# Gathered rows of expert tiles turned by VectorE in 32x32 blocks and moved on chip, in place of TensorE's transposes

## The chip, the cores and the metric

The kernel runs on one core of one Trainium2 chip. The metric is the device time of one execution in microseconds; the lower the better. A run of this kernel repeats to about 0.1%.

## The reference

Three layers follow one another, all in fp32: attention with a decay, a feed-forward layer with softplus, and a mixture of experts in which every token goes to two of eight experts. Only the last one is touched by the change.

```python
def _moe2_ref(x, w_gate, w_noise, noise, w1, w2):      # x 2304x512, w1 8x512x1024, w2 8x1024x512
    logits = x @ w_gate
    noise_scale = np.log1p(np.exp(x @ w_noise))
    noisy_logits = logits + noise_scale * noise
    top2 = np.argpartition(-noisy_logits, 2, axis=1)[:, :2]
    top2_l = np.take_along_axis(noisy_logits, top2, axis=1)
    top2_l = top2_l - top2_l.max(-1, keepdims=True)
    top2_w = np.exp(top2_l)
    top2_w /= top2_w.sum(-1, keepdims=True) + 1e-09
    out = np.zeros((N, D), dtype=np.float32)
    for e in range(E):
        for k in range(2):
            mask = top2[:, k] == e
            if not mask.any():
                continue
            h = np.maximum(x[mask] @ w1[e], 0.0)
            out[mask] += top2_w[mask, k, None] * (h @ w2[e])
    return out
```

## The kernel before

The first half of the time goes to attention and the feed-forward layer; the change leaves both alone. The expert layer then works through tiles of 128 tokens of one expert each. There are 41 tiles here, numbered g from 0, in slots s = g mod 2. How many tiles an expert has is known only when the kernel runs, so all engines read small tables (`tab`, `tab2`) with the row numbers, the expert of each tile, and whether a quarter of the next expert's weights is due in this tile.

One step g of the loop, engine by engine, in program order:

- **TensorE** (`step` in the tensor block) turns the hidden values of tile g (`hidden_transpose`, L935, 8 transposes of 128x128), computes the first product of tile g+1 (`expert_in`, 24 matmuls), turns the gathered rows of tile g+2 (`tile_transpose`, L881, 4 transposes), and computes the second product of tile g (`expert_out`, 24 matmuls). Every product is made of three matmuls (L789, L790, L791), because each operand is split into a high part and a remainder.
- **ScalarE** makes the high parts: of the hidden values (`split_hidden`, L1213, 2 instructions), of up to two quarters of weights for product one (`split_weights(g + 1, 0)`, L1226), of the turned rows (`split_tile`, L1195), the relu (L1204, L1205), and up to two quarters of weights for product two (`split_weights(g, 1)`). It also issues the small loads of the row lists (L367).
- **VectorE** makes the remainders in the same order (L1604, L1773, L1594, L1773), then scales and adds the result of tile g to the rows fetched from the output (`add_output`, L1616).
- **GpSimd** gathers the rows of tile g+3 (`gather_x`, L598), fetches the output rows of tile g (`old_rows`, L608), which waits until the rows of tile g-1 have landed, and sends the rows of tile g (`send_rows`, L614).
- **SyncE** loads a quarter of an expert's weights (1 MB, `load_raw`, L480) into `raw` as soon as VectorE has split the quarter that lay there.

Each expert but the first two has four quarters to be split, within the two or three steps around its predecessor's first tile. Experts with few tiles bring these splits close together: from 735 to 777 us of the span, three steps in a row hold eight of them.

Of the kernel before, what the change touches and what calls it, by code (L numbers as in the profile page):

```python
# [19 lines left out]
F32 = mybir.dt.float32  # L20
# [7 lines left out]
P = 128  # L28
# [82 lines left out]
def build(nc, qT, kT, kN, vN, w_ff, w_gn, noise, w_ex, c_q, c_k, c_dec, c_sq, c_small, c_pad, out):  # L111
    with ExitStack() as ctx:
# [65 lines left out]
        hE_hi, a = place("hE_hi", [P, FT2, P], F32R, a)  # L178
        hE_lo0, a = place("hE_lo0", [P, FT2 // 2, P], F32R, a)
        hE_lo1, hE_end = place("hE_lo1", [P, FT2 // 2, P], F32R, R_T + 2 * D * 4)  # L180
        assert a <= R_C and hE_end <= R_T + 2 * D * 4 + KT * P * 4
        hE_lo = (hE_lo0, hE_lo1)
# [137 lines left out]
        m1_done, relu_done, hT_made = sem("m1_done"), sem("relu_done"), sem("hT_made")  # L320
        hT_hi_done, hT_lo_done, m2_done, y_done = (sem(n) for n in ("hT_hi_done", "hT_lo_done", "m2_done", "y_done"))
# [94 lines left out]
        def _(sp):  # L416
# [108 lines left out]
            alone(sp, got_x[1], 32)  # L525
            load_weights(0, 0)
            pair = entry(sp, T_PAIR, 0, PAIR_LOW, PAIR_HIGH)

            with sp.Fori(0, pair) as i:
                for s in range(2):  # L530
                    load_weights(2 * i + s + 1, 0)
                    load_weights(2 * i + s, 1)
# [141 lines left out]
        def _(pe):  # L674
# [284 lines left out]
            def step(i, s, this, after):  # L959
                g = 2 * i + s  # L960
                hidden_transpose(g)
                expert_in(g + 1, 1 - s, *after)
                tile_transpose(g + 2, s, i + 2)
                expert_out(g, *this)
# [72 lines left out]
            tile_transpose(2 * prior + 3, 1, prior + 2)  # L1037
            expert_out(2 * prior + 1, *second, between=2 * prior + 2)
            with pe.If(two):
# [5 lines left out]
                            lambda k: hE_lo[k // 4][:, k % 4, :], y_end_ps).then_inc(m2_done, 1)  # L1045
# [9 lines left out]
        def _(act):  # L1055
# [144 lines left out]

            def relu(g):
                act.wait_ge(m1_done, g + 1)
                at_least(act, hT_made, g)
                nc.scalar.activation(hid[:, 0:512], m1_ps[0], ACT.Relu)  # L1204
                nc.scalar.activation(hid[:, 512:1024], m1_ps[1], ACT.Relu).then_inc(relu_done, 1)  # L1205
# [23 lines left out]
            def next_tile(i, s):  # L1229
                g = 2 * i + s  # L1230
                relu(g + 1)
                split_weights(g, 1)

                alone(act, sent_y[1 - s], (i + s) * 16)
                load_meta(act, meta_y, 1 - s, g + 1, ld_my[1 - s])

            def step(i, s):

                g = 2 * i + s
                alone(act, got_x[s], i * 16 + 32)  # L1240
                load_meta(act, meta_x, s, g + 4, ld_mx[s])
                split_hidden(g, g)
                split_weights(g + 1, 0)
                split_tile(g + 2, s)
                next_tile(i, s)
# [58 lines left out]

            split_hidden(2 * pair, None, hE_hi)
            with act.If(entry(act, T_TWO, 0, 0, 1)):
                split_weights(2 * pair + 1, 0)
                next_tile(pair, 0)
                split_hidden(2 * pair + 1, 2 * pair)
# [4 lines left out]
        def _(dve):  # L1314
# [285 lines left out]

            def split_hidden(g, h_hi=hT_hi, h_lo=(hT_lo[:, 0:4, :], hT_lo[:, 4:8, :])):
# [160 lines left out]
            split_second(1, 0)  # L1762
            split_second(1, 1)
# [12 lines left out]
            def step(i, s, end=False):  # L1776
# [3 lines left out]
                split_tile(g + 2, s)  # L1780
                split_weights(g, 1)
                if end:
                    split_hidden(g + 1, hE_hi, [t[:, :, :] for t in hE_lo])
# [11 lines left out]
            with dve.If(entry(dve, T_TWO, 0, 0, 1)):  # L1795
                split_weights(2 * prior + 3, 0)
                split_weights(2 * prior + 2, 1)
                split_hidden(2 * prior + 3)
# [37 lines left out]
```

## Time and profile before

| | |
|---|---|
| median of three runs | 1004.33 us (1004.1 to 1004.88) |
| profiled execution, its own time | 1005.6 us |
| its span, first to last instruction | 1003.8 us |
| TensorE busy in the span | 99% |
| VectorE, ScalarE, GpSimd busy | 40%, 42%, 20% |
| granted TensorE clock, mean | 0.999 |

The span is the stretch from the first to the last instruction, and what lies around it is 1.8 us. Shares are of the span. TensorE's busy time is that of matmuls laid over one another, so the cost of an instruction in its stream is read from the distance between starts, not from its duration.

### The profile page before, as it was taken

The page shows a single profiled execution, that of the slowest core. Times are in us where ns is not written, and L with a number is a line of the kernel's source. Part 1 is how long each engine was busy: PE and PEld are TensorE (multiplying, and loading weights), DVE is VectorE, ACT ScalarE, POOL GpSimd, SP SyncE. Part 2 cuts the span into 40 slices and gives each one's busy share as a digit, 9 for nine tenths or more (in the row PEclk, how much of TensorE's full clock was granted, in tenths as well). Part 3 has the DMA queues.
Part 4 walks back from the last instruction along what each step waited for, and adds up shares of the span by engine and source line. Part 5 has one row for each costly group of instructions (what it writes and reads, how often), then busy time and mean ns, then how long its engine had stood idle before and what let it go on. Part 6 is the DMA issues. An engine that isn't in the chain of part 4 may idle for free.

```text
span 1003.8 us, 21683 instructions
## 1 busy us (share of the span) xinstructions
PE 990.3 (99%) x5856; PEld 854.0 (85%) x5857; DVE 404.2 (40%) x803; ACT 425.3 (42%) x727; POOL 205.2 (20%) x198
## 2 busy tenths in 40 slices
PE   9899999999999999999999999999999999999997
PEld 8789998998998998989788888888888888888886
DVE  3665533432433434446563222243366464222222
ACT  2237755554555455567522222232365453222221
POOL 4540000020010200200333222222212232222222
PEclk9999999999999999999999999999999999999999
DMA  9963450000000000053316222243267451212211
GB/s 304 298 198 127 139 205 1 1 32 1 1 32 0 0 31 0 13 209 126 84 38 228 64 71 62 65 154 127 88 239 251 136 178 59 73 55 63 63 43 35
DMA packets 48380, 97.67 MB, mean 97 GB/s; under 512 B 19389, under 2 KB 24893, under 8 KB 44224
## 3 DMA queue, kind: packets, MB, share of 16 engines
q1 hardware_dynamic: 25536, 68.59, 19.8%
q0 software_dynamic: 10992, 27.84, 8.8%
q10 hardware_dynamic: 11808, 0.68, 0.8%
q8 instruction: 25, 0.41, 0.2%
q14 instruction: 19, 0.16, 0.0%
HBM read 81.31 MB, written 20.37 MB: 101 GB/s over the span
## 4 chain that ended last, share of the span: by engine, by line
PE 93%; DVE 2%; issue 2%; ACT 1%; DMA 1%; ACTq 0%; DVEq 0%; POOL 0%; POOLq 0%
PE bank L789 27%; PE bank L791 27%; PE bank L790 27%; PE bank L935 3%; PE bank L881 2%; PE bank L739 2%; PE bank L713 1%; PE bank L732 1%; PE bank L839 1%; PE bank L752 1%; PE bank L694 0%; DVE sco L1321 0%; DMA xg<-x_rows,meta_x 0%; PE bank L846 0%; DMA square<-c_sq 0%
## 5 line engine op out<-in xcount | busy, mean ns | idle before, releaser
L789 PE MATMUL bank<-ew,xgT_hi 128*128 (+1 forms) x328 | 131.5, 401 | 0.0
L789 PE MATMUL bank<-xs_hi,mw 128*128 128x384 f32 x384 | 129.9, 338 | 0.0
L791 PE MATMUL bank<-xs_hi,mw 128*128 128x384 f32 x384 | 129.5, 337 | 0.0
L790 PE MATMUL bank<-xs_lo,mw 128*128 128x384 f32 x384 | 128.9, 336 | 0.0
L789 PE MATMUL bank<-ew,hT_hi 128*128 (+1 forms) x320 | 128.3, 401 | 0.3 <-DVE hT_lo L1604 0.3
L791 PE MATMUL bank<-ew,xgT_lo 128*128 (+1 forms) x328 | 128.2, 391 | 0.0
L790 PE MATMUL bank<-ew,xgT_hi 128*128 (+1 forms) x328 | 127.8, 390 | 0.0
L791 PE MATMUL bank<-ew,hT_lo 128*128 (+1 forms) x320 | 125.1, 391 | 0.0
L790 PE MATMUL bank<-ew,hT_hi 128*128 (+1 forms) x320 | 124.8, 390 | 0.0
L789 PE MATMUL bank<-mw,g_hi 128*128 128x512 f32 x288 | 114.6, 398 | 0.0
L791 PE MATMUL bank<-mw,g_lo 128*128 128x512 f32 x288 | 113.7, 395 | 0.0
L790 PE MATMUL bank<-mw,g_hi 128*128 128x512 f32 x288 | 113.4, 394 | 0.0
L582 POOL DMA_INDIRECT lists<-rec,slot x36 | 35.7, 992 | 379.0 <-DVE slot L1482 369.9
L1383 DVE SCALAR_TENSOR_TENSOR act_t<-bank,act_t 128x384 f32<-128x384 f32 x90 | 50.2, 558 | 151.5 <-ACT act_t L1130 148.2
L1213 ACT ACTIVATE hT_hi<-bank 128x512 fp32r<-128x512 f32 x80 | 43.5, 596 | 146.5 <-PE bank L935 141.1
L614 POOL DMA_INDIRECT out<-ysb,meta_y x41 | 43.0, 1049 | 278.3 <-DVE ysb L1616 269.8
L1195 ACT ACTIVATE xgT_hi<-bank 128x512 fp32r<-128x512 f32 x42 | 25.1, 598 | 138.4 <-PE bank L881 131.7
L1126 ACT ACTIVATE act_t<-bank 128x384 f32<-128x384 f32 x90 | 44.1, 490 | 89.7 <-PE bank L791 87.8
L1616 DVE SCALAR_TENSOR_TENSOR ysb<-bank,meta_y,prev 128x512 f32<-128x512 f32 x41 | 30.7, 749 | 122.6 <-PE bank L791 97.2
L1773 DVE TENSOR_TENSOR ew<-raw,ew 128x2048 f32 x24 | 55.0, 2292 | 61.1 <-ACT ew L1226 59.4
L1594 DVE TENSOR_TENSOR xgT_lo<-bank,xgT_hi 128x512 fp32r<-128x512 f32 x42 | 29.0, 690 | 116.8 <-ACT xgT_hi L1195 112.5
L789 PEld LDWEIGHTS bank<-xs_hi,mw 128*128 128x128 f32 x384 | 72.2, 188 | 3.9
(229 smaller groups left out, 1695.5 us busy)
## 6 DMA issues: line engine op xcount, KB each, us to landing
raw<-w_ex SPq DMA_DIRECT2D x32, 1024.0 KB, 4.8
stage<-w_ff SPq DMA_DIRECT2D x16, 512.0 KB, 3.3
out<-blank SPq DMA_DIRECT2D x3, 1536.0 KB, 11.1
x_rows<-x2sb SPq DMA_DIRECT2D x6, 768.0 KB, 4.2
kbuf<-kN SPq DMA_DIRECT2D x16, 256.0 KB, 4.5
vbuf<-vN SPq DMA_DIRECT2D x16, 256.0 KB, 5.4
qbuf<-qT SPq DMA_DIRECT2D x15, 256.0 KB, 4.9
kTd<-kT SPq DMA_DIRECT2D x9, 256.0 KB, 6.4
```

What stands on the lines that cost most here:

```text
L582: pool.indirect_dma_start(out=lists[:, :], out_offset=bass.IndirectOffsetOnAxis(ap=slot[:, j, k:k + 1], axis=0), in_=rec[:, j, k, :], in_o ...
L614: pool.indirect_dma_start(out=out[:, :], out_offset=rows, in_=ysb[:, s, :], in_offset=None, bounds_check=N - 1, oob_is_err=False).then_inc ...
L789: pe.matmul(o, a_hi, b_hi, start=first, stop=False)
L790: pe.matmul(o, a_hi, b_lo, start=False, stop=False)
L791: return pe.matmul(o, a_lo, b_hi, start=False, stop=last)
L935: last = pe.transpose(hT_ps[k // 4][:, k % 4, :], hid[:, k * P:(k + 1) * P], ident)
L1126: nc.scalar.activation(t, h_ps[f % 4], ACT.Abs).then_inc(abs_done, 1)
L1213: nc.scalar.activation(h_hi[:, 4 * k:4 * k + 4, :], hT_ps[k], ACT.Copy).then_inc(hT_hi_done, 1)
L1383: dve.scalar_tensor_tensor(t, h_ps[f % 4], 0.0, t, ALU.max, ALU.add).then_inc(g_done, 1)
L1594: dve.tensor_tensor(xgT_lo[:, s, :, :], xT_ps, as32(xgT_hi[:, s, :, :]), ALU.subtract).then_inc(xgT_lo_done, 1)
L1616: dve.scalar_tensor_tensor(ysb[:, s, :], y, meta_y[:, s, 1:2].bitcast(F32), prev[:, s, :], ALU.mult, ALU.add).then_inc(y_done, 1)
L1773: dve.tensor_tensor(part(1), raw[:, w], as32(part(0)), ALU.subtract).then_inc(w_lo_done[p], 1)
```

## The change

TensorE no longer turns the gathered rows of tiles 4 and up. VectorE turns them in blocks of 32x32 (`turn_x`), three tiles ahead, into `turned_x`; SyncE moves the blocks to their partitions with four DMAs of 64 KB, in runs of 128 bytes, into `x_there` (`move_x`); ScalarE and VectorE split from there (`split_moved`) and no longer from the accumulator bank. The relu stands ahead of that split. Tiles 0 to 3 are turned by TensorE as before. The buffers of the last tile's hidden values are moved to where `raw` was, behind a wait for the last split of weights.

```diff
--- before.py
+++ after.py
@@ -175,11 +175,12 @@
         prev, a = place("prev", [P, 2, D], F32, a)
         ysb, a = place("ysb", [P, 2, D], F32, a)
         assert a <= R_C
-        hE_hi, a = place("hE_hi", [P, FT2, P], F32R, a)
-        hE_lo0, a = place("hE_lo0", [P, FT2 // 2, P], F32R, a)
-        hE_lo1, hE_end = place("hE_lo1", [P, FT2 // 2, P], F32R, R_T + 2 * D * 4)
-        assert a <= R_C and hE_end <= R_T + 2 * D * 4 + KT * P * 4
-        hE_lo = (hE_lo0, hE_lo1)
+        x_there, a = place("x_there", [P, KT, P], F32, a)
+        assert a <= R_C
+        turned_x, _ = place("turned_x", [P, D], F32, R_W - D * 4)
+        hE_hi, a = place("hE_hi", [P, FT2, P], F32R, R_X)
+        hE_lo, a = place("hE_lo", [P, FT2, P], F32R, a)
+        assert a <= R_X + 4 * QUARTER * 4
 
         square, a = place("square", [P, 2, P], F32, R_C)
         allrows, a = place("allrows", [P, P], F32R, a)
@@ -318,6 +319,7 @@
         sent_y = [sem(f"sent_y{i}") for i in range(2)]
         xgT_made, xgT_hi_done, xgT_lo_done = sem("xgT_made"), sem("xgT_hi_done"), sem("xgT_lo_done")
         m1_done, relu_done, hT_made = sem("m1_done"), sem("relu_done"), sem("hT_made")
+        x_moved = sem("x_moved")
         hT_hi_done, hT_lo_done, m2_done, y_done = (sem(n) for n in ("hT_hi_done", "hT_lo_done", "m2_done", "y_done"))
 
         def at_least(eng, s, count):
@@ -523,13 +525,32 @@
 
             sp.wait_ge(tab2_done, 1)
             alone(sp, got_x[1], 32)
+            def move_x(g):
+
+                sp.wait_ge(xgT_made, g + 1)
+                for i in range(4):
+                    sp.dma_start(x_there[:, :, 32 * i:32 * i + 32],
+                                 turned_x[32 * i:32 * i + 32, :].rearrange("a (n b) -> a n b", b=32)
+                                 ).then_inc(x_moved, 16)
+
+            def step(g, rows=True):
+                load_weights(g + 1, 0)
+                load_weights(g, 1)
+                if rows:
+                    move_x(g + 3)
+
+            sp.sem_inc(x_moved, 192)
+            move_x(4)
             load_weights(0, 0)
+            step(0, False)
+            step(1, False)
+            prior = entry(sp, T_PRIOR, 0, PAIR_LOW - 1, PAIR_HIGH - 1)
+            with sp.Fori(1, prior) as i:
+                for s in range(2):
+                    step(2 * i + s)
+            step(2 * prior)
+            step(2 * prior + 1, False)
             pair = entry(sp, T_PAIR, 0, PAIR_LOW, PAIR_HIGH)
-
-            with sp.Fori(0, pair) as i:
-                for s in range(2):
-                    load_weights(2 * i + s + 1, 0)
-                    load_weights(2 * i + s, 1)
 
             alone(sp, sent_y[0], pair * 16 + 16)
             alone(sp, sent_y[1], pair * 16)
@@ -960,7 +981,6 @@
                 g = 2 * i + s
                 hidden_transpose(g)
                 expert_in(g + 1, 1 - s, *after)
-                tile_transpose(g + 2, s, i + 2)
                 expert_out(g, *this)
 
 
@@ -1034,7 +1054,6 @@
             expert_in(2 * prior + 2, 0, *third)
             two = entry(pe, T_TWO, 0, 0, 1)
             fourth = slot_of(2 * prior + 3)
-            tile_transpose(2 * prior + 3, 1, prior + 2)
             expert_out(2 * prior + 1, *second, between=2 * prior + 2)
             with pe.If(two):
                 expert_in(2 * prior + 3, 1, *fourth)
@@ -1042,7 +1061,7 @@
             e, par = third
             pe.wait_ge(w_lo_done[1], e * 2 + 2)
             expert_out_part(2 * prior + 2, e, par, range(FT2), lambda k: hE_hi[:, k, :],
-                            lambda k: hE_lo[k // 4][:, k % 4, :], y_end_ps).then_inc(m2_done, 1)
+                            lambda k: hE_lo[:, k, :], y_end_ps).then_inc(m2_done, 1)
             with pe.If(two):
                 e, par = fourth
                 pe.wait_ge(w_lo_done[1], e * 2 + 2)
@@ -1198,6 +1217,12 @@
             split_tile(1, 1)
             keep_x2(NCH - 1)
 
+            def split_moved(g, s, done):
+
+                act.wait_ge(x_moved, g * 64)
+                act.wait_ge(m1_done, done)
+                nc.scalar.activation(xgT_hi[:, s, :, :], x_there[:, :, :], ACT.Copy).then_inc(xgT_hi_done, 1)
+
             def relu(g):
                 act.wait_ge(m1_done, g + 1)
                 at_least(act, hT_made, g)
@@ -1226,13 +1251,9 @@
                         nc.scalar.activation(ew[:, bass.ds(1 - par, 1), 0, w].rearrange("p o n -> p (o n)"),
                                              raw[:, w], ACT.Copy).then_inc(w_hi_done[p], 1)
 
-            def next_tile(i, s):
-                g = 2 * i + s
-                relu(g + 1)
-                split_weights(g, 1)
-
+            def next_rows(i, s):
                 alone(act, sent_y[1 - s], (i + s) * 16)
-                load_meta(act, meta_y, 1 - s, g + 1, ld_my[1 - s])
+                load_meta(act, meta_y, 1 - s, 2 * i + s + 1, ld_my[1 - s])
 
             def step(i, s):
 
@@ -1241,8 +1262,10 @@
                 load_meta(act, meta_x, s, g + 4, ld_mx[s])
                 split_hidden(g, g)
                 split_weights(g + 1, 0)
-                split_tile(g + 2, s)
-                next_tile(i, s)
+                relu(g + 1)
+                split_moved(g + 2, s, g + 1)
+                split_weights(g, 1)
+                next_rows(i, s)
 
             def split_second(p, q):
 
@@ -1302,10 +1325,12 @@
                 for s in range(2):
                     step(i, s)
 
+            for p in range(2):
+                act.wait_ge(w_lo_done[p], 2 * E)
             split_hidden(2 * pair, None, hE_hi)
             with act.If(entry(act, T_TWO, 0, 0, 1)):
-                split_weights(2 * pair + 1, 0)
-                next_tile(pair, 0)
+                relu(2 * pair + 1)
+                next_rows(pair, 0)
                 split_hidden(2 * pair + 1, 2 * pair)
             alone(act, ld_mx[1], pair * 16 + 32)
 
@@ -1598,6 +1623,17 @@
             split_tile(1, 1)
             keep_x2(NCH - 1)
 
+            def turn_x(s, count):
+
+                dve.wait_ge(got_x[s], count * 16)
+                dve.transpose(turned_x[:, :].rearrange("p (j c b) -> p j c b", j=4, b=32),
+                              xg[:, s, :].rearrange("p (c a j) -> p j c a", j=4, a=32)).then_inc(xgT_made, 1)
+
+            def split_moved(g, s):
+                dve.wait_ge(xgT_hi_done, g + 1)
+                dve.tensor_tensor(xgT_lo[:, s, :, :], x_there[:, :, :], as32(xgT_hi[:, s, :, :]), ALU.subtract
+                                  ).then_inc(xgT_lo_done, 1)
+
             def split_hidden(g, h_hi=hT_hi, h_lo=(hT_lo[:, 0:4, :], hT_lo[:, 4:8, :])):
                 for k in range(2):
                     dve.wait_ge(hT_hi_done, 2 * g + k + 1)
@@ -1760,6 +1796,7 @@
             split_tile(3, 1)
             add_output(0, 1, False)
             split_second(1, 0)
+            turn_x(0, 3)
             split_second(1, 1)
 
             def split_weights(g, p):
@@ -1777,10 +1814,12 @@
                 g = 2 * i + s
                 split_hidden(g)
                 split_weights(g + 1, 0)
-                split_tile(g + 2, s)
+                split_moved(g + 2, s)
                 split_weights(g, 1)
                 if end:
-                    split_hidden(g + 1, hE_hi, [t[:, :, :] for t in hE_lo])
+                    split_hidden(g + 1, hE_hi, (hE_lo[:, 0:4, :], hE_lo[:, 4:8, :]))
+                else:
+                    turn_x(1 - s, i + s + 2)
                 add_output(i, s)
 
             dve.wait_ge(tab_done, 1)
@@ -1793,8 +1832,6 @@
             step(prior, 1, True)
 
             with dve.If(entry(dve, T_TWO, 0, 0, 1)):
-                split_weights(2 * prior + 3, 0)
-                split_weights(2 * prior + 2, 1)
                 split_hidden(2 * prior + 3)
             dve.wait_ge(got_prev[0], entry(dve, T_PREV, 0, PAIR_LOW, PAIR_HIGH + 1) * 16)
             add_output(prior + 1, 0, y=y_end_ps)
```

## Rows read from the trace of the kernel before

**Rows 1.** Page, part 1: busy us of each engine, share of the span, instructions.

```profile
PE 990.3 (99%) x5856; PEld 854.0 (85%) x5857; DVE 404.2 (40%) x803; ACT 425.3 (42%) x727; POOL 205.2 (20%) x198
```

**Rows 2.** Stretches: from:to, length, busy PE, PEld, DVE, ACT, POOL, clock, DMA, GB/s.

```profile
735.00:777.00 42.00, 41.75 (x204) 34.51 (x203) 27.87 (x24) 23.27 (x24) 9.19 (x10) 1.00 0.73 259
```

**Rows 3.** Timeline of TensorE: start, us, engine, line, operation, count, idle before.

```profile
764.80 0.49 PE L789 MATMUL bank<-ew,hT_hi 128*128 x1 [0.25 <-DVE hT_lo L1604]
```

**Rows 4.** Line L881, 535 to 989 us: duration ns min/median/max, starts.

```profile
L881 PE MATMUL bank<-square,xg x148: 270/273/275, 543.3 to 985.4; 128*128 128x128 f32 x148
```

**Rows 5.** Timeline of TensorE around one tile's four transposes.

```profile
788.79 0.40 PE L791 MATMUL bank<-ew,xgT_lo 128*128 x1
789.03 0.60 PE L881 MATMUL bank<-square,xg 128*128 128x128 f32 x4
789.38 0.48 PE L789 MATMUL bank<-ew,hT_hi 128*128 x1
789.70 0.39 PE L790 MATMUL bank<-ew,hT_hi 128*128 x1
789.93 0.40 PE L791 MATMUL bank<-ew,hT_lo 128*128 x1
```

**Rows 6.** Line L1728: VectorE's turn of two blocks of 32x32.

```profile
L1728 DVE STREAM_TRANSPOSE tab<-cols x1: 233/233/233, 511.0 to 511.0; 32x64 int32<-32x64 int32 x1
```

**Rows 7.** Timeline of SyncE's queue: loads issued, 745 to 765 us.

```profile
745.56 18.37 SPq L480 DMA_DIRECT2D raw<-w_ex  x5
```

**Rows 8.** Line L480, the loads of weights, over the span.

```profile
DMA to landing us min/median/max: 4.7/4.8/7.5
```

**Rows 9.** DMA queues, 64.2 to 64.78 us: packets, MB, share of 16 engines.

```profile
q1 hardware_dynamic: 481, 0.06, 65.4%
```

**Rows 10.** Line L455: one load of 64 KB in 512 runs of 128 bytes.

```profile
L455 SPq DMA_DIRECT2D wg<-w_gn x1: 435/435/435, 63.2 to 63.2; - x1
...
DMA to landing us min/median/max: 2.1/2.1/2.1
```

**Rows 11.** Timeline of VectorE, 743 to 788 us.

```profile
743.07 2.29 DVE L1773 TENSOR_TENSOR ew<-raw,ew 128x2048 f32 x1 [1.33 <-issue]
...
746.75 2.29 DVE L1773 TENSOR_TENSOR ew<-raw,ew 128x2048 f32 x1 [0.79 <-ACT ew L1226]
...
761.11 2.29 DVE L1773 TENSOR_TENSOR ew<-raw,ew 128x2048 f32 x1 [0.52 <-ACT ew L1226]
...
770.62 2.29 DVE L1773 TENSOR_TENSOR ew<-raw,ew 128x2048 f32 x1 [0.36 <-issue]
...
775.97 1.28 DVE L1604 TENSOR_TENSOR hT_lo<-bank,hT_hi 128x512 fp32r<-128x512 f32 x2
...
786.65 1.28 DVE L1604 TENSOR_TENSOR hT_lo<-bank,hT_hi 128x512 fp32r<-128x512 f32 x2
```

**Rows 12.** Timeline of ScalarE: splits of gathered rows, 752 to 778 us.

```profile
752.33 0.60 ACT L1195 ACTIVATE xgT_hi<-bank 128x512 fp32r<-128x512 f32 x1
...
766.80 0.57 ACT L1195 ACTIVATE xgT_hi<-bank 128x512 fp32r<-128x512 f32 x1
...
777.40 0.60 ACT L1195 ACTIVATE xgT_hi<-bank 128x512 fp32r<-128x512 f32 x1 [4.58 <-PE bank L881]
```

**Rows 13.** Timeline of VectorE, 671 to 689 and 807 to 824 us.

```profile
671.73 2.29 DVE L1773 TENSOR_TENSOR ew<-raw,ew 128x2048 f32 x1 [2.00 <-ACT ew L1226]
...
687.81 1.28 DVE L1604 TENSOR_TENSOR hT_lo<-bank,hT_hi 128x512 fp32r<-128x512 f32 x2
...
807.29 2.29 DVE L1773 TENSOR_TENSOR ew<-raw,ew 128x2048 f32 x1 [1.87 <-ACT ew L1226]
...
822.92 1.28 DVE L1604 TENSOR_TENSOR hT_lo<-bank,hT_hi 128x512 fp32r<-128x512 f32 x2
```

**Rows 14.** Timeline of ScalarE: splits of gathered rows, 678 and 814 us.

```profile
678.81 0.60 ACT L1195 ACTIVATE xgT_hi<-bank 128x512 fp32r<-128x512 f32 x1 [4.61 <-PE bank L881]
...
814.17 0.60 ACT L1195 ACTIVATE xgT_hi<-bank 128x512 fp32r<-128x512 f32 x1 [1.09 <-PE bank L881]
```

## The prediction

> **What bounds the kernel now.** I read three views. The page's busy times first: TensorE is busy for 990.3 of 1003.8 us, and no other engine reaches half of that [rows 1]. So whatever leaves TensorE's stream is a gain, if nothing else becomes late. Then the busy times by stretch: even where the weight splits are densest, TensorE is busy for 41.75 of 42 us, while VectorE is busy for 27.87 and the DMA engines for 73% of the time [rows 2]. Last TensorE's timeline: its one wait among the tiles lies there, 0.25 us for VectorE's hidden remainder [rows 3]. The reader is to see that TensorE bounds every tile, and that in this stretch the next bound is already level with it.
>
> **What leaves TensorE.** Outside tiles 0 to 4, 148 transposes are recorded [rows 4], 37 tiles of four; tile 4's go too, so 38 tiles lose theirs. The price is read from starts. From the last matmul of the first product (788.79) to the second matmul of the next (789.70) are 0.91 us; two ordinary distances (789.70 to 789.93, 0.23 each) would be 0.45. So a tile's transposes cost 0.46 us, 38 of them 17.5 us. Bounds: 0.36 us (the distance 789.03 to 789.38, 13 us in all) and 0.60 us (the recorded duration, 23 us); I take the distances, since only they show when the next matmul starts. A tile's period is half of 764.80 to 789.38, 12.29 us [rows 3, 5], and becomes 11.8.
>
> **What is added, and where it lies.** VectorE gets one turn a tile. The trace has none over 512 elements a partition. An ordinary operation over so many takes half of 1.28 us, 0.64 [rows 11]; a turn of two blocks took 0.233 us [rows 6], and eight times that is 1.9. I take 0.8, near the first, because at the ordinary rate the 64 columns are 0.08 of those 0.233 us, and the rest is paid once; 0.6 and 1.9 stay as bounds. The turn stands behind the splits of the step and ahead of `add_output` and the next tile's hidden remainder. It needs the gather of tile g+3, which GpSimd issues behind the rows sent of tile g-1, at the step's beginning; I cost that wait at nothing, and if the gather were late, `add_output` and TensorE's next product for want of its bank would be behind it. VectorE is busy for 404.2 of 1003.8 us [rows 1], and less in a light step, so there the 0.8 us are hidden. ScalarE's split reads SBUF in place of a bank; I cost that, the changed order of relu and split, and the new places of the last buffers at nothing (0.1 us a tile either way; ScalarE has slack in light steps, and the last weights are split over 100 us before the end).
>
> SyncE gets four DMAs a tile behind the loads of weights of the same step, and on the same queue. The moved rows are needed by ScalarE one step later, and behind that split stands ScalarE's split of weights for product two. This makes a loop from tile to tile: split of weights (ScalarE, VectorE), load, turn, move, split of rows, split of weights. How long is its DMA part? The load is issued 0.2 us after VectorE frees the quarter (743.07 + 2.29 = 745.36 against 745.56, [rows 7, 11]) and lands 4.8 us after that [rows 8]. The move is behind it in the queue. Its price: in 0.58 us 481 packets of 128 bytes filled 65.4% of 16 engines [rows 9], 12.6 ns each, so 2048 packets are 1.6 us of each engine. Lag from VectorE's split to the rows being there: 0.2 + 4.8 + 1.6 = 6.6 us.
>
> The Trainium skill (DMA: Bandwidth & Descriptors, Queues, rings and completion order) says that each DMA engine takes the descriptors of one queue in ring order; no run here shows two such DMAs apart. The same page (Why small descriptors are slow) says that 128-byte packets between SBUF and SBUF still reach 78% of the link, which with its 435 GB/s would make the move 0.8 us, an estimate, and the lag 5.8; its first table asks for 512 bytes or more for full rate, which the 12.6 ns for 128 bytes agree with. By the 0.8 us the sum below would be some 5 us better.
>
> In a light step nothing is loaded and the lag is well under a tile. Where a split for product two is followed one tile later by another, the time that was there is that from VectorE's end to ScalarE's split of rows: 749.04 to 752.33 = 3.3; 763.40 to 766.80 = 3.4; 772.91 to 777.40 = 4.5 [rows 11, 12]; 674.02 to 678.81 = 4.8; 809.58 to 814.17 = 4.6 [rows 13, 14]; the link one tile after this last one is taken as equal. Missing against 6.6: 3.3, 3.2, 2.1, 1.8, 2.0 and 2.0 us. They add up within a cluster, because the loop itself is later each time. To them come 0.8 for the turn and 0.46 for each tile by which TensorE is early; off goes the slack, from the first half of the hidden remainder to TensorE's first matmul on it: 690.8 - 688.4 = 2.4 (690.8 is 764.80 less 0.25 and six periods), 0 at 764.80, 777.1 - 776.6 = 0.5, 789.4 - 787.3 = 2.1, 826.2 - 823.6 = 2.6 (826.2 is three periods after 789.38) [rows 3, 5, 11, 13].
> - First cluster: 1.8 + 0.8 + 0.5 - 2.4 = 0.7.
> - Second: 3.3 + 0.8 + 1.4 - 0 = 5.5 at the first link, 6.5 + 0.8 + 1.8 - 0.5 = 8.6 at the second, 8.6 + 0.8 + 2.3 - 2.1 = 9.6 at the third; the last counts, 9.6.
> - Third: 2.0 + 0.8 + 0.9 - 2.6 = 1.1, then 4.0 + 0.8 + 1.4 - 2.6 = 3.6.
>
> TensorE waits 13.9 us that it did not wait before. Sum: 17.5 - 13.9 = 3.6 us faster. The profiled execution took 1005.6 us (span 1003.8 and 1.8 around it), so it would be 1002.0; against the median of 1004.33 that is 1000.7.
>
> **Rivals.**
> - The move is not held up by the load, or the loop has more room than I count. Then the lag is 0.8 (turn) + 0.2 + 2.1 + 3 x 0.44 for three more issues [rows 10] = 4.4 us. Missing: 1.1, 1.0, 0, and 0 elsewhere. Second cluster: 2.1 + 0.8 + 1.8 - 0.5 = 4.2 us, the others nothing: 13.3 us faster, 991.0. For it speaks that the rings hold little at any time (73% at the densest); against it, that loads and moves share one queue.
> - The loop becomes the bound outright: slower. Its point of decision is the lag, and it is 7.2 us, since each further us costs one in each of six links and 3.6 are to be used up. The same window shows 19.3 ns from packet to packet on an engine (0.58 x 16 / 481), so the move may take 2.5 us, and a DMA's fixed part (2.1 less 0.6) may come on top: lag 7.5 to 9.0. At 8.2 the six links cost 9.6 us more, 6.0 us slower than before: 1010.3. At 9.0 it is some 1016. For it: TensorE's one wait and the 73% of the DMA engines lie in just this stretch. Against it: descriptors can be laid out while the load runs.
> - The turn itself costs its upper bound, 1.9 us: 1.1 more in each of three clusters, 3.3 us, 1004.0, no change.
>
> **How the numbers follow.** This kernel's measurement tells 0.2%, or 2 us, from no change: below 1002.3 is faster, above 1006.3 slower. My forecast (lag 6 to 7.2) has 0.42, of which 0.23 faster, 0.12 no change, 0.07 slower, by the spread of the slacks; the first rival 0.25; the slow one 0.30; the third 0.03, put to no change with 0.02 and to slower with 0.01. Faster 0.48, no change 0.14, slower 0.38. The range takes in the first rival with a few us beyond it and the slow one up to a lag of 8.7: 987 to 1014. The likeliest case alone is 997 to 1005.
>
> **What would show each step.** Light steps: TensorE's period 11.8 us, no L881 after tile 3, hidden turn of 0.6 to 1.0 us. Second cluster: ScalarE's split of rows waiting for a DMA at three tiles in a row, TensorE idle 3 to 6 us before the first matmul on the hidden values, waiting for VectorE, 10 us in all. The packets of the move: 1.6 us, starting where those of the load end. Wrong would be: no waits for the moved rows (first rival), or waits in light steps as well, for which I have no term.

## The result, and the profile after

The changed kernel took 1021.69 us (median of 4, 1020.58 to 1021.93) against 1004.22 (1003.01 to 1004.88) for the kernel before on the same chip: ratio 1.0173, interval 1.016 to 1.0187. It is slower, where 1000.7 us was forecast. The spans of the profiled executions are 1019.6 and 1003.8 us, 15.8 apart. One of the four executions of e7 below took 1380.76 us at a granted clock of 0.65; its median and ratio are those of the other three.

Part 1 of its page answers [rows 1]; below it three rows of the list of waits (engine, line waited for: us in all, times, longest).

```profile
PE 983.7 (96%) x5704; PEld 844.6 (83%) x5705; DVE 443.8 (44%) x841; ACT 427.2 (42%) x727; POOL 207.7 (20%) x198
```

```profile
ACT xgT_hi L1224 <- DMA x_there<-turned_x: 42.7, 12, 11.4
PE bank L810 <- DVE hT_lo L1640: 16.9, 8, 5.2
PE bank L810 <- DVE xgT_lo L1634: 7.6, 1, 7.6
```

152 transposes fewer, but only 6.6 us less TensorE time, and TensorE now waits. Its timeline has every wait among the tiles; in place of the one of [rows 3] there are nine, the eight below and one of 0.96 us at 530.42:

```profile
556.49 0.79 PE L810 MATMUL bank<-ew,xgT_hi 128*128 x1 [7.62 <-DVE xgT_lo L1634]
...
696.59 0.50 PE L810 MATMUL bank<-ew,hT_hi 128*128 x1 [1.98 <-DVE hT_lo L1640]
...
758.02 0.50 PE L810 MATMUL bank<-ew,hT_hi 128*128 x1 [1.77 <-DVE hT_lo L1640]
...
775.25 0.79 PE L810 MATMUL bank<-ew,hT_hi 128*128 x1 [5.18 <-DVE hT_lo L1640]
...
804.38 0.54 PE L810 MATMUL bank<-ew,hT_hi 128*128 x1 [2.67 <-DVE hT_lo L1640]
...
843.88 0.49 PE L810 MATMUL bank<-ew,hT_hi 128*128 x1 [2.24 <-DVE hT_lo L1640]
...
857.86 0.49 PE L810 MATMUL bank<-ew,hT_hi 128*128 x1 [1.92 <-DVE hT_lo L1640]
...
871.77 0.49 PE L810 MATMUL bank<-ew,hT_hi 128*128 x1 [0.22 <-DVE hT_lo L1640]
```

The three clusters forecast are there, with 2.0, 9.6 and 4.4 us (forecast: 0.7, 9.6, 3.6). Not forecast are the 8.6 us at the start. Why some of these matmuls last 0.79 us and not 0.49 is in the stretches (columns as in [rows 2]; the eighth is the granted clock), and in TensorE's timeline behind the first wait:

```profile
540.00:560.00 20.00, 12.38 (x51) 9.88 (x51) 2.44 (x3) 2.26 (x5) 1.38 (x2) 0.80 0.53 175
...
580.00:650.00 70.00, 70.00 (x334) 58.41 (x333) 22.92 (x30) 16.14 (x30) 18.32 (x18) 1.00 0.36 89
770.00:790.00 20.00, 14.82 (x59) 12.03 (x59) 13.28 (x13) 7.79 (x11) 3.63 (x4) 0.83 0.70 228
880.00:1000.00 120.00, 120.00 (x571) 100.08 (x571) 39.37 (x52) 27.27 (x51) 32.58 (x32) 1.00 0.36 86
```

```profile
557.51 0.63 PE L812 MATMUL bank<-ew,xgT_lo 128*128 x1
557.93 0.63 PE L810 MATMUL bank<-ew,xgT_hi 128*128 x1
558.36 0.63 PE L811 MATMUL bank<-ew,xgT_hi 128*128 x1
```

The matmuls start 0.43 us apart instead of 0.23: TensorE ran at 1.2 GHz in four stretches (552.1 to 562.3, 774.0 to 780.8, 804.7 to 808.1, 859.3 to 862.7), each in or behind a wait. Of the time worked there (the stretch less the wait in it) 0.20 / 0.43 is lost: 2.7 + 2.6 + 1.6 + 1.6 = 8.5 us. In the light steps, 580 to 650 and 880 to 1000, the clock is 1.00, TensorE never waits, and a tile takes 11.8 us, as forecast. So: 17.5 gone, 24.3 us of waits (24.6 less the 0.25 of before) and 8.5 at the low clock added, +15.3 of the +15.8 us between the profiled executions. By the medians the change costs 17.4 us; the 1.6 us between the two are not explained.

Now the first cause of the waits, on SyncE's queue, at the start and in the densest cluster:

```profile
527.41 2.77 SPq L532 DMA_DIRECT2D x_there<-turned_x  x4
532.29 13.78 SPq L482 DMA_DIRECT2D raw<-w_ex  x4
550.53 9.98 SPq L532 DMA_DIRECT2D x_there<-turned_x  x6
...
756.67 2.82 SPq L532 DMA_DIRECT2D x_there<-turned_x  x4
762.74 10.68 SPq L482 DMA_DIRECT2D raw<-w_ex  x3
773.91 2.71 SPq L532 DMA_DIRECT2D x_there<-turned_x  x4
```

At the start 23 us lie between the move of tile 4 and that of tile 5. The chain of waits says what they are (530 to 556 us, shares by line):

```profile
by line: SPq L360 33.2%; issue 23.2%; SPq L482 10.5%; SPq L532 10.0%; DMA x_there<-turned_x 9.1%; SPq L356 8.4%; DVE xgT_lo L1634 2.7%; ACT xgT_hi L1224 2.5%; SPq L520 2.4%; SPq L523 0.6%; SPq L548 0.4%; SPq L530 0.2%
```

L360 and L356 are table reads, with which SyncE decides for each half of a product's weights whether there is a load. The move of tile 5 is behind seven such calls, 20.3 us together, of which four parts load anything: not the loads' bytes hold it, but SyncE itself. In the dense cluster the loop is the one described: VectorE's split ends at 755.65 (753.36 + 2.29), the move follows, and ScalarE's split of the rows starts at 762.55, a lag of 6.9 us.

```profile
753.36 2.29 DVE L1810 TENSOR_TENSOR ew<-raw,ew 128x2048 f32 x1 [2.98 <-ACT ew L1251]
755.57 1.07 DVE L1629 STREAM_TRANSPOSE turned_x<-xg 128x512 f32<-128x512 f32 x1
```

```profile
762.55 0.63 ACT L1224 ACTIVATE xgT_hi<-x_there 128x512 fp32r<-128x512 f32 x1 [2.77 <-DMA x_there<-turned_x]
```

The load was issued at 755.87, before the move (756.67 above). The packets show the order that the prediction gave: none under 512 bytes from 756 to 760 us, and from 760 to 762.25 all 2048 of the move, with some 120 of 4 or 8 bytes:

```profile
DMA packets 122, 1.00 MB, mean 250 GB/s; under 512 B 0, under 2 KB 0, under 8 KB 0
```

```profile
DMA packets 2214, 0.48 MB, mean 211 GB/s; under 512 B 2168, under 2 KB 2168, under 8 KB 2208
```

But the load is only a small part of the lag. At the last tile of the last cluster none goes ahead of the move, and the lag, from 869.39 to 875.24, is still 5.8 us: 1.0 for the turn, 2.7 for the issue of the four moves, 2.1 from there to the split.

```profile
867.10 2.29 DVE L1810 TENSOR_TENSOR ew<-raw,ew 128x2048 f32 x1 [4.44 <-ACT ew L1251]
```

```profile
875.24 0.63 ACT L1224 ACTIVATE xgT_hi<-x_there 128x512 fp32r<-128x512 f32 x1 [2.56 <-DMA x_there<-turned_x]
```

### The profile page after: what moved, and what is told of

The parts are those of the page before. It is cut to its first block, busy times and chain, and to the rows that moved or that the text cites. A ratio compares the mean times of both kernels' runs of the same rounds, so it can differ in the third digit from the quotient of the medians.

```text
span 1019.6 us, 21595 instructions
## 1 busy us (share of the span) xinstructions
PE 983.7 (96%) x5704; PEld 844.6 (83%) x5705; DVE 443.8 (44%) x841; ACT 427.2 (42%) x727; POOL 207.7 (20%) x198
## 4 chain that ended last, share of the span: by engine, by line
PE 77%; issue 5%; SPq 4%; ACTq 4%; DMA 3%; ACT 3%; DVE 3%; DVEq 1%; POOL 0%; POOLq 0%
PE bank L810 23%; PE bank L812 23%; PE bank L811 23%; DMA x_there<-turned_x 3%; PE bank L956 2%; SPq L532 2%; ACT ew L1251 2%; PE bank L760 2%; ACTq L360 2%; PE bank L734 2%; ACTq L356 1%; SPq L360 1%; PE bank L753 1%; DVE ew L1810 1%; PE bank L860 1%
## 5 line engine op out<-in xcount | busy, mean ns | idle before, releaser
L1634 DVE TENSOR_TENSOR xgT_lo<-x_there,xgT_hi 128x512 fp32r<-128x512 f32 x38 | 26.3, 692 | 149.4 <-ACT xgT_hi L1224 145.1
L810 PEld LDWEIGHTS bank<-ew,hT_hi 128*128 128x128 f32 x320 | 61.5, 192 | 32.9 <-issue 20.3
L810 PEld LDWEIGHTS bank<-ew,xgT_hi 128*128 128x128 f32 x328 | 62.3, 190 | 20.5 <-issue 8.9
```

Of the source, the lines that this page charges most:

```text
L810: pe.matmul(o, a_hi, b_hi, start=first, stop=False)
L1634: dve.tensor_tensor(xgT_lo[:, s, :, :], x_there[:, :, :], as32(xgT_hi[:, s, :, :]), ALU.subtract).then_inc(xgT_lo_done, 1)
```

## The experiments

Theory T: the added time is waits for moved rows that stand behind SyncE's load calls, at the start and in the loop, and the half rate behind long waits. Rival C: the moves' packets slow whatever shares the DMA engines. Rival D: VectorE's added work is the price. "Against before" is (ratio - 1) x 1004.2 us, since the runs were made in several lots with the kernel before beside each. Of the code of each only the main lines are shown; "..." stands for what is left out.

| kernel | median us | ratio, 95% interval | against before |
|---|---|---|---|
| the change | 1021.69 | 1.0173 [1.016, 1.0187] | +17.4 |
| e1 start order | 1018.35 | 1.0153 [1.0133, 1.0173] | +15.4 |
| e2 move first | 1014.98 | 1.0116 [1.0099, 1.0133] | +11.6 |
| e3 + turn early | 1010.82 | 1.0075 [1.0058, 1.0092] | +7.5 |
| e5 = e1 + e3 | 1007.52 | 1.0027 [1.0013, 1.0041] | +2.7 |
| e14 gather early alone | 1020.81 | 1.0175 [1.0158, 1.0192] | +17.6 |
| e8b = e5 + gather early | 995.06 | 0.9919 [0.9897, 0.9941] | -8.1 |
| e16 = e8b + tile 6 early | 993.46 | 0.9902 [0.9886, 0.9919] | -9.8 |
| e18 = e16, coarse moves | 995.48 | 0.9912 [0.9893, 0.9931] | -8.8 |
| e12 coarse moves | 1017.45 | 1.0133 [1.0109, 1.0157] | +13.4 |
| e4 turns, moves unused | 1011.44 | 1.0079 [1.0055, 1.0103] | +7.9 |
| e9 turns unused | 1005.02 | 1.0011 [1.0002, 1.0021] | +1.1 |
| e6 fill of 56 | 1028.61 | 1.0242 [1.0221, 1.0263] | +24.3 |
| e6b fill of 28 | 1020.26 | 1.0171 [1.0153, 1.0189] | +17.2 |
| e7 moves by ScalarE | 1038.82 | 1.034 [1.0319, 1.036] | +34.1 |
| e8 = e7 + both early | 1023.81 | 1.0188 [1.0166, 1.0211] | +18.9 |
| e10 moves by GpSimd | 1086.11 | 1.081 [1.0791, 1.0828] | +81.3 |

### SyncE's order at the start

```diff
             move_x(4)
+            move_x(5)
             load_weights(0, 0)
             step(0, False)
             step(1, False)
+            step(2, False)
+            step(3)
...
-            with sp.Fori(1, prior) as i:
+            with sp.Fori(2, prior) as i:
```

> SyncE issues the moves of tiles 4 and 5 before it loads the third expert's weights; the loop is as changed. Theory T (the added time is waits for moved rows that stand behind weight loads on SyncE, some at the start and some in the loop, and half-rate TensorE after them): the 7.6 us wait at 556 us and the 2.7 us at the low clock behind it go, so 1021.7 - 7.6 - 2.7 = 1011.4 us, 9 to 11 us below the changed kernel; the waits of the clusters (16 us) stay. Theory C (the short packets of the moves slow everything that shares the DMA engines): no order changes that, 1020 to 1023 us.

Half right: the wait for tile 5 is gone, but one of 5.24 us for tile 6 took its place at 565.64. In this kernel (e1) tile 6's move was issued at some 560 us, again behind SyncE's calls, so that the removal of one wait uncovered the next. What the start gave, the clusters took back: TensorE's waits sum to 24.7 us, as in the change (24.6). The gain lies in the time lost at half rate, 5.0 us instead of 8.5.

### The order in the loop: move before the load, turn before the split

```diff
                 load_weights(g + 1, 0)
-                load_weights(g, 1)
                 if rows:
                     move_x(g + 3)
+                load_weights(g, 1)
```

> In SyncE's loop the move stands before the load of the second product's weights, not behind it; start and VectorE as changed. Theory T: the cluster waits (16.0 us) are set by a turn-to-split lag of 6.9 us, of which the load ahead in the queue is some 1.6 to 4; without it the lag is 4.5 to 5.3 and most of the cluster waits go, with the 5.8 us of low clock behind them, the start stays: 1021.7 - 10 to 20, about 1007 us. Rival D (the lag is the turn and the copy themselves): no change, 1020 to 1023. Theory C: the same as D, 1020 to 1023.

5.7 us less (e2): neither D nor C, which expected none, but less than T's 10 to 20, and not where T had it. The cluster from 767 to 865 us still has eight waits, the longest 4.51, and the waits behind the start sum to 15.3 us against 16.0, although no lag in that cluster is longer than 6.1 us (6.5 to 7.7 in the change where a load went ahead). The gain is at the start, 6.3 us of waits instead of 8.6, since one call fewer stands ahead of tile 5's move, and in the time lost at half rate, 4.1 us instead of 8.5. The load now stands behind the four issues; whether that takes the shorter lag back is not shown.

```diff
                 split_moved(g + 2, s)
+                if not end:
+                    turn_x(1 - s, i + s + 2)
                 split_weights(g, 1)
...
```

> As the kernel with the move first, and VectorE turns the tile before it splits the second product's weights, so neither that split nor its load stands in the loop from moved rows to the next move. Theory T: no cluster wait is left (the loop's length falls far below a tile's TensorE time), the start's waits of 8.6 us and its 2.7 us of low clock stay: 1021.7 - 16 - 5.8 = about 999.9 us. Rival D (work added to VectorE is the price, wherever it stands): 1018 to 1023. Theory C: 1018 to 1023.

4.1 us less again (e3), 7.5 over the kernel before where T had foretold 4 below it. VectorE's and GpSimd's timelines show what came late next:

```profile
776.86 1.08 DVE L1629 STREAM_TRANSPOSE turned_x<-xg 128x512 f32<-128x512 f32 x1 [5.50 <-DMA xg<-x_rows,meta_x]
```

```profile
769.44 2.22 POOL L619 DMA_INDIRECT xg<-x_rows,meta_x  x1 [0.30 <-issue]
```

The early turn asks for rows whose gather GpSimd has just issued, behind the output rows of the tile before. In the changed kernel VectorE waited 2.5 us in all for gathers; here 34.5.

> The start's order (tiles 4 and 5 moved before the third expert's loads) and the early turn with the move first, together. If the two savings add, as theory T has it (waits on one path at different places): 1010.8 - 3.3 = 1007.5 us. If a wait that both leave (the fourth expert's loads ahead of tile 6's move) sets the start in both, only the loop's part counts: 1010 to 1011 us.

They add, as far as the intervals tell: 1007.5 us as forecast (e5), though by the ratios it is 14.7 us off the change, against 2.0 and 9.8 alone. The start's wait was 3.60 us.

### The gather one tile earlier

```diff
             def step(i, s):
-                gather_x(1 - s, i + s + 2, 2 * i + s + 2)
                 old_rows(s, i + 1, (i + s) * 16)
+                gather_x(s, i + 3, 2 * i + s + 3)
                 send_rows(s, 2 * i + s + 1)
...
```

> The kernel with both orders changed (start, early turn, move first; 1007.5 us), and GpSimd fetches each tile's rows one tile earlier, behind the fetch of old rows. There VectorE stood 31 us waiting for gathered rows. If the gather is what the early turn runs into, and so what holds the dense stretch: the waits of 9 us after 750 us mostly go, 998 to 1002 us. If the ring of stored and fetched output rows, and the loads that it shares the DMA engines with, hold it: 1006 to 1010 us.

10.8 us less by the ratios (e8b), faster than the kernel before and below the 998 to 1002 expected. VectorE's waits for gathers are gone. Is it the gather by itself?

> The changed kernel with the one edit that GpSimd fetches each tile's rows a tile earlier. Added to the kernel with both orders it brought 12.5 us. If it helps only where the turn is early (in the changed kernel VectorE waits 2.5 us in all for gathered rows, and the moves are held by SyncE's queue): 1020 to 1023 us. If the earlier gather is itself what gained, in any order: 1008 to 1012 us.

No: alone on the changed kernel it brings nothing (1.0175 against 1.0173), its waits being those of the change to within a us or two. So this edit's gain is not its own; each bound was hidden by the one before it: SyncE's queue, then VectorE's turn, then the gather.

### The rest of the start's wait, and the number of small runs

```diff
             step(1, False)
+            move_x(6)
             step(2, False)
-            step(3)
+            step(3, False)
```

> The fastest kernel so far (both orders, gather a tile earlier; 995.1 us), and SyncE moves tile 6 before, not behind, the last three of its calls at the start that load weights. There SyncE needed 19.7 us from the move of tile 5 to that of tile 6, nearly all of it table reads. If these reads are the start's wait of 3.35 us: 995.1 - 3.3 = 991.8 us. If tile 7's move takes its place: 994 to 996 us.

The wait went from 3.35 to 0.85 us; median 993.46, the lowest here, between the two forecasts, though the intervals do not tell e16 from e8b. SyncE's queue, then TensorE's busy time in two stretches, the first that of [rows 2]:

```profile
526.82 9.90 SPq L532 DMA_DIRECT2D x_there<-turned_x  x8
538.83 13.36 SPq L482 DMA_DIRECT2D raw<-w_ex  x4
552.24 20.28 SPq L532 DMA_DIRECT2D x_there<-turned_x  x10
```

```profile
735.00:777.00 42.00, 38.89 (x182) 31.30 (x181) 28.50 (x25) 22.48 (x25) 13.82 (x11) 1.00 0.81 254
540.00:560.00 20.00, 20.00 (x97) 16.41 (x95) 3.73 (x5) 4.36 (x8) 5.09 (x5) 1.00 0.85 287
```

```profile
560.91 0.49 PE L814 MATMUL bank<-ew,xgT_hi 128*128 x1 [0.85 <-DVE xgT_lo L1638]
...
745.08 0.50 PE L814 MATMUL bank<-ew,hT_hi 128*128 x1 [1.17 <-DVE hT_lo L1644]
758.28 0.49 PE L814 MATMUL bank<-ew,hT_hi 128*128 x1 [1.15 <-DVE hT_lo L1644]
```

Its waits sum to 5.3 us, and no stretch among the tiles is at half clock. Its profiled span is 990.4: 1003.8 - 17.5 + 5.1 = 991.4. In the profiled executions the 17.5 us of the forecast are thus there once little waits. By the ratio e16 is 9.8 us faster than the kernel before and not 12.4: the profiled execution before was 1.3 us above its median, this one 1.2 us below. That rest is not explained.

In two kernels a move is four copies of 32 runs of 2 KB instead of 512 of 128 bytes (the rows stay in wrong partitions):

```diff
-                    sp.dma_start(x_there[:, :, 32 * i:32 * i + 32],
-                                 turned_x[32 * i:32 * i + 32, :].rearrange("a (n b) -> a n b", b=32)
...
+                    sp.dma_start(x_there[32 * i:32 * i + 32, :, :].rearrange("p k m -> p (k m)"),
+                                 turned_x[32 * i:32 * i + 32, :]).then_inc(x_moved, 16)
```

> The changed kernel with each move's 2048 runs of 128 bytes replaced by 128 runs of 2 KB (four instructions, the same bytes, queue and order; the rows so moved stay in the wrong partitions, so the result of the experts' products is left out). If the runs' number decides (2.75 us issue and 2.3 us landing in the lag of 6.9 us): the lag falls by 3 to 4 us, the clusters go, the start's wait stays but for 2 us: 1001 to 1004 us. If the place behind the loads decides alone: 1016 to 1020 us.

> The kernel with all orders changed, with each move's 2048 runs of 128 bytes replaced by 128 runs of 2 KB (rows stay in the wrong partitions, so the experts' products aren't those of the reference). If the small runs still cost in the dense stretch, through the output rows' ring that shares the DMA engines (waits of some 4.5 us there): 3 to 5 us below the kernel with real moves. If they are hidden: within 1.5 us of it.

In the changed kernel 16 times fewer runs (e12) bring 4.0 us of 17.4, as "the place decides" had it (1016 to 1020); four such issues still take 2.4 us of SyncE, against 2.7. In the best kernel they bring nothing (e18, 0.9912 against 0.9902, intervals overlap). Rival C fails as the main cause: its part in the change is at most these 4 us.

### The added work with its result unused

Both kernels let TensorE turn the tiles as before and read its result. The first (e4) adds turns and moves, the second (e9) turns alone. In the first, VectorE must also wait for the move before it overwrites what is moved:

```diff
+                dve.wait_ge(x_moved, (2 * count + s - 3) * 64)
...
+                tile_transpose(g + 2, s, i + 2)
```

> All turns and moves are made as in the change, but their result is left unused: TensorE turns the gathered tiles as before, and both splits read its result. Theory T (only the wait for moved rows costs): TensorE's work is that of before, 1004.2, plus at most 2 us where the 1.1 us turn on VectorE stands in dense steps: 1004 to 1007 us. Theory C (queue, packets or memory traffic slow the other work): the added time is there without the waits for moved rows: 1004.2 + 8 to 33, so 1012 us or more.

> Only the turns are added (38 of 1.09 us on VectorE), their result is unused and nothing is moved; TensorE turns the tiles as before. The kernel with unused turns and moves took 7.6 us over the kernel before. If the turn on VectorE (with its wait for gathered rows, ahead of the output addition) is what that paid: 1008 to 1012 us. If the moves' packets and queue are: 1003.5 to 1006 us.

Turns alone: +1.1 us, so rival D falls (1.09 us a turn, 38 of them, nearly all hidden). With moves +7.9, between 5.5 and 10.3: more than T allowed, and at the lower edge of what C asked (8 us). Two things are in it: VectorE waits 14.1 us for moves by the wait that this kernel adds itself, and in the dense stretch the fetch of old output rows is late. VectorE and GpSimd there:

```profile
779.86 0.75 DVE L1659 SCALAR_TENSOR_TENSOR ysb<-bank,meta_y,prev 128x512 f32<-128x512 f32 x1 [5.88 <-issue]
```

```profile
771.00 2.85 POOL L630 DMA_INDIRECT prev<-out,meta_y  x1 [2.52 <-DMA out<-ysb,meta_y]
```

TensorE waits 1.28 us behind the longer of VectorE's waits (9.74 us), 2.86 us behind the late fetch, and runs at half rate for 3.4 us behind that; the issue of this fetch is one of the long ones of the last section. So the profile puts the larger part on the fetch. What made the rows late beyond the long issue, the moves' packets or something else, stays open.

### Is it the clock?

28 or 56 unused products on TensorE inside the start's wait:

```diff
             step(1, 1, early[1], early[2])
+            for _ in range(56):
+                pe.matmul(gate_ps[:, 0:P], ident, ident, start=True, stop=True)
```

> The changed kernel with 56 unused 128x128 products on TensorE (6.3 us at their spacing in the fill, L700, of some 0.11 us) inside the 7.6 us wait at the start, so that it is not idle there; nothing else differs and the wait itself stays. If the half-rate matmuls from 552 to 562 us come of the idleness: they are gone, 1021.7 - 2.7 = 1019.0 us, granted clock 1.00 there. If the clock falls for another reason: 1021 to 1023 us.

Mis-sized (e6): each product is two instructions, 12.66 us in all, which overran the wait; 1028.6 us. The clock was 1.00 through the fill, but a wait of 2.1 us was left behind it, and from 563.0 to 566.4 TensorE ran at half rate.

> As the kernel with unused products in the start's wait, with 28 of them: each made two instructions of 0.113 us, so these take 6.3 us, less than the wait of 7.6. If idleness alone drops the clock: no stretch at half rate after the start's wait, 1021.7 - 2.7 = 1019.0 us. If not: 1021 to 1023 us.

Stretches of the changed kernel, then of this one (e6b):

```profile
546.00:556.00 10.00, 2.87 (x17) 2.12 (x15) 0.34 (x1) 0.63 (x1) 0.00 (x0) 0.80 0.49 138
556.00:566.00 10.00, 9.51 (x30) 7.62 (x31) 3.38 (x5) 2.11 (x5) 3.06 (x3) 0.68 0.34 81
```

```profile
546.00:556.00 10.00, 8.26 (x66) 7.77 (x65) 0.69 (x1) 0.63 (x1) 1.00 (x1) 1.00 0.50 154
556.00:566.00 10.00, 10.00 (x49) 8.41 (x49) 3.71 (x5) 2.69 (x5) 3.06 (x3) 1.00 0.38 88
```

49 matmuls in place of 30 in the same 10 us. The third output addition behind the wait starts at 579.67 instead of 582.20, 2.5 us earlier (2.7 expected). At the last tile 1.3 of them are left, and the ratios don't tell the two kernels apart: the later clusters took the rest back. That idleness drops the clock is shown; that mending it alone pays is not, and neither is which waits drop it: in the change the wait of 1.92 us at 857.86 was followed by half rate, that of 2.24 us at 843.88 was not. The Trainium skill (TensorE: Matmul & The Clock Gate, Part 1) names the same two levels, chosen by how busy the engine has been; the rows agree.

### The moves on another engine's queue

```diff
                 split_hidden(g, g)
+                move_x(g + 2)
                 split_weights(g + 1, 0)
                 relu(g + 1)
```

> The changed kernel with the four moves of a tile issued by ScalarE, after its split of the hidden rows, instead of by SyncE behind the weight loads; turns where the change has them. Theory Q (the added time is the place of the moves in SyncE's order, behind loads and their table reads): the start's 8.6 us and most of the 16 us in the loop go, with the 8.5 us of low clock: 1021.7 - 25 to 33, that is 989 to 997 us, below the kernel before. Theory R (the moves are late wherever they are issued, since the turn is late on VectorE, or ScalarE's 2.6 us of issue per tile makes its own splits late): 1005 to 1020 us.

Beyond both ranges (e7). The moved rows are in time (ScalarE waits for a move twice, 5.8 us in all), but ScalarE is now late itself. ScalarE's timeline, then TensorE's:

```profile
744.44 2.71 ACTq L1213 DMA_DIRECT2D x_there<-turned_x  x4
750.56 1.91 ACT L1248 ACTIVATE ew<-raw 128x2048 f32 x1 [7.94 <-issue]
```

```profile
756.39 1.97 PE L946 MATMUL bank<-square,hid 128*128 128x128 f32 x8 [4.78 <-ACT hid L1227]
```

The issue of four moves holds ScalarE's queue for 2.7 us, with its own table reads around them; the split of weights and, behind it in order, the relu come too late for TensorE, whose waits sum to 36.0 us. 42% busy said nothing of that, since the issuing of DMAs and table reads isn't counted as busy.

> As the kernel with ScalarE's moves, and VectorE turns a tile right behind the split of the moved rows, and GpSimd fetches each tile's rows one tile earlier, behind the fetch of old rows. With the turn early and SyncE's moves, VectorE stood 34.5 us waiting for gathered rows. Theory G (the gather was what the early turn ran into): no wait of VectorE for gathered rows, 987 to 996 us. If instead the ring of stored and fetched output rows is the tightest in the dense stretch, the waits there stay: 996 to 1004 us.

Wrong too (e8). No wait of VectorE for gathered rows is left, as theory G had it, and the kernel is 15 us better than its base; but TensorE still waits 26.8 us, and ScalarE's queue holds 10% of the chain that ended last (7% in the base, 4% in the change). That this queue is what bounds it is read from the chain, and not tested by a run.

```diff
                 gather_x(1 - s, i + s + 2, 2 * i + s + 2)
+                move_x(2 * i + s + 2)
                 old_rows(s, i + 1, (i + s) * 16)
```

> The changed kernel with the four moves of a tile issued by GpSimd, between the fetch of gathered rows and the fetch of old rows, instead of by SyncE behind the weight loads. Theory Q (what the moves stand behind decides): GpSimd idles some 11 us of each tile, so the moves are early, the start's wait goes and the clusters' too: 990 to 1000 us if its issue of four moves stays under some 4 us. If the issue takes longer than 8 us a tile, the ring of stored and fetched output rows becomes the bound: 1030 us and more.

GpSimd's timeline in a light step, and ScalarE's wait:

```profile
583.15 3.03 POOL L630 DMA_DIRECT2D x_there<-turned_x  x4
```

```profile
ACT xgT_hi L1222 <- DMA x_there<-turned_x: 180.5, 38, 8.9
```

The issue took 3.0 us, under the 4 that I had named as harmless, and yet it is the worst kernel (e10): here the move comes after the output rows are sent, so ScalarE waits for it in every one of 38 tiles, TensorE's waits for the remainders sum to 58.6 us, and twelve stretches at half rate take more. Where a queue stands in time decided here, and not how idle its engine was.

## Why the prediction was wrong

- What leaves TensorE (17.5 us, tile 11.8): right; period 11.8 in the light steps, and the best kernel's span shows the whole sum.
- The turn (0.8): 1.09 us measured, within the bounds, hidden in light steps.
- The loop in the clusters (lag 6.6, 13.9 us of waits): places right, and the move's packets start where the load's end, as forecast; size 16.0, with a lag of 6.9 where read. That would have left 1002.8 us. The closeness is in part luck: the four issues, 2.7 to 2.9 us of SyncE, stand in no term of the lag of 6.6, and behind the turn and them the load ahead adds only 1.1 us (6.9 against 5.8). The move's packets took 13 ns each, as taken, but 2.2 us together instead of 1.6, and the 0.8 us worked out beside that did not show.
- The first rival (lag 4.4): with no load ahead the lag was still 5.8, since an issue of a move took 0.63 us and not 0.44.
- **The step that failed: "In a light step nothing is loaded and the lag is well under a tile."** At the start the steps are light for VectorE, but SyncE runs behind with calls of `load_weights`, seven of them with 2.9 us each between the two moves. I had counted the moves' wait for loads and not SyncE's own time, and had not laid out the order of its queue for tiles 5 and 6: 8.6 us of waits. The signs of being wrong named this case: waits where the forecast had no term.
- **A term that was missing: the clock.** I had priced a wait at its length. Behind four waits 8.5 us more were lost at half rate. In the profile before the clock is 1.00 among the tiles, so no row could show it; a forecast that adds waits of several us to an engine never idle needs a margin for it.
- The slow rival (1010 to 1016) had the right sign and too small a size, since it too was a lag in the clusters alone; no rival held the start. Its sum for a lag of 9.0 is 1015.1 and not 1016.
- The gather costed at nothing: right in the changed kernel (2.5 us on VectorE), wrong as soon as the turn was early.
- Together: 1000.7 + 2.1 for the clusters + 8.6 for the start + 8.5 for the clock = 1019.9 of 1021.7 us.

## What to carry to other kernels

Work moved from the bound engine to DMA is worth its full price only if the whole ring (fetch, turn, move, split) is ahead of the engine by a tile at every point, the start included; write down each in-order queue past which the move is issued, with its register and table reads, which no busy time shows. Mending one link shows the next, so an edit that brings nothing alone (the earlier gather) may bring 10 us after the others. And a wait on TensorE can cost more than itself: that of 7.6 us cost 2.7 more, that of 5.2 cost 2.6.

## What the runs showed of the hardware

Indirect DMAs on GpSimd mostly take 1.0 us to issue, but up to 3.1 (e3) where the issue begins while VectorE subtracts two operands in SBUF. GpSimd's and VectorE's timelines of the changed kernel:

```profile
759.52 2.93 POOL L619 DMA_INDIRECT xg<-x_rows,meta_x  x1 [0.31 <-issue]
```

```profile
759.25 2.29 DVE L1810 TENSOR_TENSOR ew<-raw,ew 128x2048 f32 x1 [0.79 <-ACT ew L1251]
```

The issue ends at 762.45, 0.9 us after VectorE's split (761.54). Two such issues in the clusters of the change and eleven behind 640 us in the best kernel end 0.9 us after a subtraction of weights or of moved rows; beside a turn alone none is stretched. The kernel before has two of them behind 640 us (2.72 us at 803.0, 1.38 at 828.5). The change adds a kind, since the remainder of the rows is now taken from two operands in SBUF and no longer from a bank: two of the eleven (1.35 and 1.29 us) end behind it, the others behind a subtraction of weights. The Trainium skill (GPSIMD Engine Reference, Key points) says that GpSimd's SBUF interfaces contend with VectorE instructions of two SBUF inputs; the trace agrees, with these 0.9 us.
